# Masks of both tiles as signs from ScalarE in a top-k attention with a gated product

## The chip, the cores and the metric

The kernel runs on one core of one Trainium2 chip. The metric is device microseconds of that core, the median of several runs. Lower is better. Engines are named as in the profile: PE is TensorE (PEld its weight loads), ACT is ScalarE, DVE is VectorE, POOL is GpSimd, SP is SyncE, which issues most DMAs. All times are microseconds (us) unless marked ns.

## What is computed

Attention over 4 x 8 heads with 576 rows of 64 columns. Each row of scores keeps only its 32 largest entries; the others are masked before the softmax. The result, 2304 tokens of 512 columns, then goes through a gated product of two matrices and an output matrix.

```python
B, H, S, D = q.shape          # 4, 8, 576, 64
scores = (1.0 / np.sqrt(D)) * np.matmul(q, k.transpose(0, 1, 3, 2))
kth = np.partition(scores, -32, axis=-1)[..., -32:-31]
scores = np.where(scores >= kth, scores, -1000000000.0)
scores = scores - np.max(scores, axis=-1, keepdims=True)
attn = np.exp(scores)
attn = attn / (np.sum(attn, axis=-1, keepdims=True) + 1e-09)
attn_out = np.matmul(attn, v)
x = attn_out.transpose(0, 2, 1, 3).reshape(B * S, H * D)
out = (x @ w_a) * (x @ w_b) @ w_out   # 512 -> 1536 -> 512
```

## The kernel before

**Units.** The attention is cut into 72 units. A unit is 128 query rows of two heads (a pair), or, for the last 64 rows of the sequence, 64 rows of each of four heads (a tail unit). Its scores are two tiles, j = 0 and 1, of 128 x 576 float32, in `scores[:, u % 3, j, :]`. Four units make the 128 tokens of a group, 18 groups in all. The gated product of a group is made in four chunks of 384 of the 1536 inner columns, so there are 72 chunks too, and chunk n runs in step s = n + 5. All products are made of high and low parts (three matmuls for one), which is why copies, differences and `_hi`, `_lo` tiles are everywhere.

**Steps.** Each engine runs a hand-written program with a loop over steps s, and semaphores tie the programs together. Nothing is reordered: an engine that waits holds all that is written behind it. In step s a unit is in each stage of a pipeline:

- PE: `probs_v(s-2)` (L557), scores of unit s+1 (`qk`, L523), half of the columns of chunk n (L588), transposition of the hidden tile (`turn_hidden`, L599), nine transpositions of the normalised scores of unit s-1 (`transposes`, L539: four for tile 0, five for tile 1), transposed keys and queries, `output(n-2)` (L620), the other half of the columns of chunk n (L588). For each first chunk of a group (n % 4 == 0) a part of the first half is made behind the transpositions (`late_blocks`).
- ACT: in this order `exps(s-1)` for both tiles (L724, two ACTIVATEs with sums), `guard` (L732, the sums plus epsilon), in one of four steps `copy_y` (L793), `x_out(s-2)` (L759, L762), `copy_ab(n-1, 1)` (L773), the scores of unit s+1 out of PSUM (L702, two halves) with `normalise(s-1)` (L739) behind each half, `copy_probs_t(s-1)` (L747, L749), `mask_sign(s)` (L715), `copy_q(s+3)` (L692, L694), `copy_hidden(n-1)` (L780, L782), `copy_ab(n, 0)` (L773, in the first chunk of a group it stands behind the guard of the next step instead), and in 12 steps (four for each of the batches 1 to 3: steps 10, 12, 15, 16, 28, 30, 32, 34, 46, 48, 51, 52) `copy_k` (L678, L682), the keys of a coming pair.
- POOL: `negate(s-1)` (L882), which makes `neg`, the negated scaled maximum and the negated scaled 32nd value of each row, from `best`; `masked(s-1, 0)` and `masked(s-1, 1)` (L901), which add `keep` to the scores; `split_k` (L866) in the steps of keys; `hidden_lo(n-2)` (L917), `hidden(n-1)` (L908), `low_of_x`, `split_q`.
- DVE: the search for the 32 largest of both tiles of unit s. Four rounds of MAX8 (`find`, L976), with MATCH_REPLACE8 between them (`take_out`, L993). The reciprocal of the sums of unit s-1 (`invert`, L1003) stands behind the second `take_out`. At the unit's end comes the comparison with the 32nd value, `below` (L1008), which writes -3e38 where a score is lower and 0 elsewhere into `keep[:, j, :]`.

**Two ways to a mask.** In units 0 to 9 DVE compares for both tiles. From unit 10 (`SIGN0`) it compares for tile 0 alone, and ACT makes the mask of tile 1: `mask_sign` takes the sign of (score - 32nd value) as int8 into the highest byte of each float of `keep`, which held -3e38. A negative sign gives a byte of all ones, so the float is about -3e38 again; 0 and +1 give a float near zero. A memset in unit 10 (L1031) sets the floats up once, and `s_keep` tells ACT of it. The addition on POOL waits for `keep_ready[j]`.

Of the kernel before, what the change touches and what calls it, by code (L numbers as in the profile page):

```python
# [6 lines left out]
def topk_attention_gated_product(nc, q, k, v, w_parts, xs, out):  # L7
    fp32, fp32r, int8 = mybir.dt.float32, mybir.dt.float32r, mybir.dt.int8
    ALU, ACT = mybir.AluOpType, mybir.ActivationFunctionType

    P = 128
    BH, S, D = q.shape
    TOPK = 32
    ROUNDS = TOPK // 8
    SCALE = 1.0 / D ** 0.5
    NEG = -3.0e38
# [32 lines left out]
    ROWS = 3  # L49
# [35 lines left out]
    for n in range(KB, NPREPS):  # L85
        b, p, old = n // KB, n % KB, n - KPAIRS
# [52 lines left out]
    with ExitStack() as ctx:  # L139
        def sb(name, shape, dt=fp32):  # L140
            return ctx.enter_context(nc.sbuf_tensor(name, shape, dt))

        def sem(name):
            return ctx.enter_context(nc.semaphore(name))
# [16 lines left out]
        scores = sb("scores", [P, ROWS, 2, S])  # L161
        work = sb("work", [P, 2, S])
        keep = sb("keep", [P, 2, S])
        best = sb("best", [P, 2, 2, TOPK])

        neg = sb("neg", [P, 2, 2, 2])
# [14 lines left out]

        keep_sign = keep[:].rearrange("p j c -> p (j c)").bitcast(int8).rearrange("p (j c b) -> p j c b", j=2, b=4)[:, 1, :, 3]

        ps = ctx.enter_context(nc.psum_tensor("ps", [P, 8, 512], fp32))

# [65 lines left out]
        s_keep = sem("s_keep")  # L253
# [28 lines left out]
        keep_ready = [sem("keep0_ready"), sem("keep1_ready")]  # L282
        mask_done = sem("mask_done")
# [24 lines left out]
        def unit(u):  # L308
            return 0 <= u < NU
# [347 lines left out]
        def _(act):  # L657
            A = nc.scalar
# [5 lines left out]
            def weights(s, m):  # L664
                for i in w_of(s, m):
                    split_hi(i)
# [38 lines left out]
                act.wait_ge(qk_done, 2)  # L705
                A.copy(scores[:, 0, j, :].rearrange("p (a c) -> p a c", a=2), ps[:, j:j + 3:2, 0:HALF]).then_inc(s_ready, 1)  # L706

            def mask_sign(u):
                if not unit(u) or u < SIGN0:
                    return  # L710
                act.wait_ge(neg_ready, u + 1)
                if u == SIGN0:
                    act.wait_ge(s_keep, 1)
                act.wait_ge(mask_done, 2 * (u - 1) + 2)
                A.activation(keep_sign, scores[:, u % ROWS, 1, 0:S], ACT.Sign, bias=neg[:, u % 2, 1, 1:2], scale=SCALE  # L715
                             ).then_inc(keep_ready[1], 1)

            def exps(u, j):
                if not unit(u):
# [31 lines left out]
            def x_out(u):  # L751
                if not unit(u):
                    return
                b, t, pairs, place = UNITS[u]
                g, at = columns(u)
                act.wait_ge(pv_done, u + 1)
                if g >= 2:
                    wait(act, ab_done[1], NH * (g - 1))
                A.copy(x_hi[:, g % 2, pairs[0]:pairs[-1] + 1, at:at + P // len(pairs)],  # L759
                       ps_x.rearrange("p (j c) -> p j c", j=len(pairs))).then_inc(xhi_done, 1)  # L760
                wait(act, xlo_done, u)
                A.copy(x_raw[:], ps_x).then_inc(xraw_done, 1)  # L762
# [41 lines left out]
            for s in range(FIRST, MOE_END):  # L804
                n = s - MOE0
                if s == NU:
                    x_out(s - 2)
                exps(s - 1, 0)
                exps(s - 1, 1)
                guard(s - 1)  # L810
                if late_blocks(n - 1):
                    copy_ab(n - 1, 0)
                if s >= NU:
                    copy_ab(n - 1, 1)
                if s != NU + 2:
                    copy_y(n - 3)
                weights(s, 0)
                if s != NU:
                    x_out(s - 2)
                if s < NU:  # L820
                    copy_ab(n - 1, 1)
                copy_scores(s + 1, 0)
                weights(s, 1)
                normalise(s - 1, 0)
                copy_scores(s + 1, 1)
                weights(s, 2)
                normalise(s - 1, 1)
                copy_probs_t(s - 1, 0)
                copy_probs_t(s - 1, 1)
                mask_sign(s)  # L830
                copy_q(s + 3)
                weights(s, 3)
                copy_hidden(n - 1)
                if not late_blocks(n):
                    copy_ab(n, 0)
                for m in preps_at(s):
                    copy_k(m)
                weights(s, 4)
                if s == NU + 1:
                    copy_y(n - 2)  # L840
# [105 lines left out]
        @block.vector  # L946
        def _(dve):
            V = nc.vector
            count = 1

            V.memset(k_rows[TAIL:P, :, FULL, :, :], 0.0).then_inc(s_kpad, 1)
            V.memset(work[:], 0.0).then_inc(chain, 1)
            dve.wait_ge(chain, 1)
            for n in range(2):
                V.tensor_copy(q_t[:, n, :, :], work[:, :, 0:6 * D]).then_inc(s_qzero, 1)
            dve.wait_ge(qhi_ready, 1)
            dve.wait_ge(q_copied, 1)
            V.tensor_tensor(q_columns(0, 1), q_whole[:].rearrange("p (b c) -> p b c", b=2), q_columns(0, 0),
                            ALU.subtract).then_inc(qt_ready, 1)
            dve.wait_ge(khi_ready, 1)  # L960
            V.tensor_tensor(k_t[:, 0, 1, :], keys_in_psum(0)[0][0][:, 0:S], k_t[:, 0, 0, :], ALU.subtract
                            ).then_inc(klo_first, 1)
            for h in range(2):
                rows = slice((1 - h) * TAIL, (2 - h) * TAIL)
                ins = V.memset(v_rows[rows, :, TAILS, h * D:(h + 1) * D], 0.0)
            ins.then_inc(s_vpad, 1)

            def find(u, r):
                nonlocal count
                for j in range(2):  # L970
                    if r > 0:
                        dve.wait_ge(chain, taken[j])
                    elif u == 0:
                        dve.wait_ge(s_ready, j + 1)
                    src = scores[:, u % ROWS, j, 0:S] if r == 0 else work[:, j, :]
                    ins = V.max(best[:, u % 2, j, 8 * r:8 * r + 8], src)  # L976
                    if r == ROUNDS - 1:
                        ins.then_inc(kth_ready, 1)
                    elif r == 0:
                        ins.then_inc(max_ready, 1)  # L980
                    else:
                        ins.then_inc(chain, 1)
                        count += 1
                        found[j] = count

            def take_out(u, r, j):
                nonlocal count
                src = scores[:, u % ROWS, j, 0:S] if r == 0 else work[:, j, :]
                if r == 0:
                    dve.wait_ge(max_ready, 2 * u + j + 1)  # L990
                else:
                    dve.wait_ge(chain, found[j])
                V.match_replace(out=work[:, j, :], in_to_replace=best[:, u % 2, j, 8 * r:8 * r + 8],  # L993
                                in_values=src, imm_value=NEG).then_inc(chain, 1)
                count += 1
                taken[j] = count

            def invert(u):
                if not unit(u):
                    return  # L1000
                dve.wait_ge(eps_ready, u + 1)
                wait(dve, p_ready, 2 * (u - 2) + 2)
                V.reciprocal(inverse[:, u % 2, :], sums_eps[:]).then_inc(inv_ready, 1)  # L1003

            def below(u, j):
                dve.wait_ge(kth_ready, 2 * u + j + 1)
                wait(dve, mask_done, 2 * (u - 1) + j + 1)
                V.tensor_scalar(keep[:, j, :], scores[:, u % ROWS, j, 0:S], best[:, u % 2, j, TOPK - 1:TOPK], NEG,  # L1008
                                ALU.is_lt, ALU.mult).then_inc(keep_ready[j], 1)

            found, taken = [0, 0], [0, 0]
            for s in range(NU):
                if s > 0:
                    dve.wait_ge(s_ready, 2 * s + 2)
                find(s, 0)
                take_out(s, 0, 0)
                take_out(s, 0, 1)
                find(s, 1)
                take_out(s, 1, 0)
                take_out(s, 1, 1)  # L1020
                invert(s - 1)
                find(s, 2)
                take_out(s, 2, 0)
                take_out(s, 2, 1)
                find(s, 3)
                below(s, 0)
                if s < SIGN0:
                    below(s, 1)
                elif s == SIGN0:
                    dve.wait_ge(mask_done, 2 * s)  # L1030
                    V.memset(keep[:, 1, :], NEG).then_inc(s_keep, 1)  # L1031
            invert(NU - 1)

# [28 lines left out]
```

## Time and profile before

| | |
|---|---|
| median of 3 runs | 818.16 us (817.97 to 818.72) |
| the profiled execution's own time | 817.8 us |
| its span, first to last instruction | 815.4 us |
| PE busy | 771.7 us (95%) |
| DVE busy | 744.3 us (91%) |
| ACT busy | 657.0 us (81%) |
| POOL busy | 507.4 us (62%) |
| mean granted PE clock | 0.98 |

Busy time is the time in which at least one instruction of the engine runs. A matmul is pipelined and its end is modelled: one of 384 columns is listed with some 340 ns and the next starts about 175 ns after it. So a busy PE may still have short holes, and starts say more than durations. ACT and DVE instructions overlap a little too. A bracket behind a row of the timeline is the idle time of the engine before that instruction, and what ended it.

### The profile page before, as it was taken

The numbers are of one execution on the slowest core, as the hardware profiler recorded it, in microseconds if no ns is written. First come the engines' busy times: TensorE is split into PE (matmuls) and PEld (weight loads), VectorE is DVE, ScalarE is ACT, GpSimd is POOL, SyncE is SP. The second block draws the span as 40 slices with busy tenths as digits, with TensorE's granted clock in tenths as the row PEclk, the third lists the DMA queues.
The fourth block names the chain that finished last, engine by engine and source line by source line (L and its number), as shares of the span: only waits on it lengthen the run. The fifth ranks groups of instructions, "written<-read, shape, count | busy, mean of one in ns | idle before, by whom it ended". The sixth has DMA issues, their size and how long they took to land.

```text
span 815.4 us, 18431 instructions
## 1 busy us (share of the span) xinstructions
PE 771.7 (95%) x5952; PEld 686.3 (84%) x5952; DVE 744.3 (91%) x1603; ACT 657.0 (81%) x1614; POOL 507.4 (62%) x560
## 2 busy tenths in 40 slices
PE   5368899999999999999999999999999999999998
PEld 4246788899998989898889899989998889898887
DVE  6999999998999999999999999999999999999500
ACT  5678978888888888888888888888888888888732
POOL 2989986656555666666756565665656555665532
PEclk9957999999999999999999999999999999999999
DMA  6566754445553444444644443544463434343562
GB/s 169 150 186 199 217 185 148 138 137 150 149 167 113 140 125 129 126 138 142 178 142 134 128 137 122 145 136 136 137 183 123 137 124 137 124 133 117 167 214 84
DMA packets 117245, 119.16 MB, mean 146 GB/s; under 512 B 61856, under 2 KB 80288, under 8 KB 117152
## 3 DMA queue, kind: packets, MB, share of 16 engines
q1 hardware_dynamic: 116880, 117.93, 47.8%
q8 instruction: 50, 0.82, 0.4%
q14 instruction: 43, 0.35, 0.2%
q10 hardware_dynamic: 272, 0.07, 0.0%
HBM read 108.53 MB, written 9.44 MB: 145 GB/s over the span
## 4 chain that ended last, share of the span: by engine, by line
PE 86%; POOL 5%; DVE 4%; DMA 2%; issue 2%; ACT 1%; SPq 0%; POOLq 0%; ACTq 0%
PE ps L588 37%; PE ps L620 18%; PE ps L557 10%; PE ps L523 9%; PE ps L539 8%; PE ps L599 3%; DVE best L976 2%; DVE work L993 2%; POOL scores L901 2%; POOL w_lo L856 1%; POOL k_t L856 1%; DMA x_scratch<-k_t 1%; PE ps L492 1%; PE ps L501 1%; DMA stage<-in_w 0%
## 5 line engine op out<-in xcount | busy, mean ns | idle before, releaser
L976 DVE MAX8 best<-work 128x8 f32<-128x576 f32 x432 | 304.4, 747 | 0.0
L901 POOL TENSOR_TENSOR scores<-scores,keep 128x576 f32<-128x576 f32 x144 | 207.0, 1441 | 37.4 <-ACT keep L715 36.6
L993 DVE MATCH_REPLACE8 work<-best,work 128x576 f32<-128x576 f32 x288 | 212.0, 745 | 0.0
L588 PE MATMUL ps<-w_hi,x_hi 128*128 128x384 f32 x576 | 202.5, 351 | 2.4 <-issue 1.2
L588 PE MATMUL ps<-w_hi,x_lo 128*128 128x384 f32 x576 | 194.4, 338 | 0.0
L908 POOL TENSOR_TENSOR ab<-ab 128x384 f32<-128x384 f32 x72 | 73.3, 1018 | 158.6 <-ACT ab L773 158.6
L588 PE MATMUL ps<-w_lo,x_hi 128*128 128x384 f32 x432 | 145.8, 337 | 0.0
L747 ACT COPY probs_t<-ps 128x512 f32<-128x512 f32 x144 | 82.2, 586 | 51.8 <-PE ps L539 49.7
L588 PEld LDWEIGHTS ps<-w_hi,x_hi 128*128 128x128 f32 x576 | 108.1, 188 | 17.5 <-issue 13.9
L724 ACT ACTIVATE scores<-scores,neg 128x576 f32<-128x576 f32 x144 | 114.4, 822 | 6.6 <-POOL scores L901 6.4
L739 ACT ACTIVATE scores<-scores,inverse 128x576 f32<-128x576 f32 x144 | 115.4, 803 | 0.3 <-DVE inverse L1003 0.3
L539 PE MATMUL ps<-ident,scores 128*128 128x128 f32 x648 | 90.1, 283 | 26.2 <-ACT scores L702 19.2
L588 PEld LDWEIGHTS ps<-w_hi,x_lo 128*128 128x128 f32 x576 | 108.1, 188 | 0.0
L993 DVE MATCH_REPLACE8 work<-best,scores 128x576 f32<-128x576 f32 x144 | 106.0, 745 | 0.0
L976 DVE MAX8 best<-scores 128x8 f32<-128x576 f32 x144 | 101.9, 750 | 2.5 <-ACT scores L706 2.5
L539 PEld LDWEIGHTS ps<-ident,scores 128*128 128x128 f32 x648 | 74.7, 145 | 33.5 <-ACT scores L739 17.8
L557 PE MATMUL ps<-probs_t,v_rows 128*64 128x128 f32 (+1 forms) x1600 | 99.5, 274 | 2.5 <-ACT probs_t L749 2.5
L557 PEld LDWEIGHTS ps<-probs_t,v_rows 128*64 128x64 f32 x1600 | 82.3, 141 | 21.0 <-issue 16.9
L702 ACT COPY scores<-ps 128x576 f32<-128x576 f32 x142 | 93.4, 658 | 2.0 <-PE ps L523 1.9
L620 PE MATMUL ps<-w_hi,h_hi 128*128 128x512 f32 x216 | 91.1, 422 | 0.5 <-issue 0.4
L523 PE MATMUL ps<-k_t,q_t 64*128 64x288 f32 x960 | 87.6, 319 | 3.3 <-ACT k_whole L682 1.9
L588 PEld LDWEIGHTS ps<-w_lo,x_hi 128*128 128x128 f32 x432 | 81.3, 188 | 3.0
(64 smaller groups left out, 1300.9 us busy)
## 6 DMA issues: line engine op xcount, KB each, us to landing
wo_lo<-x_scratch SPq DMA_DIRECT2D x69, 768.0 KB, 4.5
wb_lo<-x_scratch SPq DMA_DIRECT2D x70, 384.0 KB, 4.1
stage<-in_w SPq DMA_DIRECT2D x36, 256.0 KB, 3.1
x_scratch<-k_t SPq DMA_DIRECT2D x18, 256.0 KB, 2.4
k_rows<-in_k SPq DMA_DIRECT2D x32, 128.0 KB, 4.7
v_rows<-in_v SPq DMA_DIRECT2D x32, 128.0 KB, 2.6
out<-stage SPq DMA_DIRECT2D x16, 256.0 KB, 4.2
q_rows<-in_q SPq DMA_DIRECT2D x63, 64.0 KB, 3.5
```

Of the source, the lines that this page charges most:

```text
L523: last = mm(ps_s[half][:, j, :], q_t[rows, u % 2, qpart, first:first + 2 * D], k_t[rows, (b * KB + p) % KPAIRS, kpart, at:at + HALF], star ...
L539: last = tr(to, row_of(u)[:, at:at + P], ident[:])
L557: last = mm(ps_x[h * D:(h + 1) * D, i * w:(i + 1) * w], v_rows[:, p, block, h * D:(h + 1) * D], probs_t[:, at:at + w], start=(i == 0 and c ...
L588: last = mm(ps_ab[which], x[:, g % 2, kb, :], w, start=(kb == 0 and m == 0), stop=(kb == KB - 1 and m == 2))
L620: last = mm(ps_y, x[:, cols], w, start=(f + b == 0 and m == 0), stop=(f + b == NF - 1 and m == 2))
L702: A.copy(scores[:, u % ROWS, :, half * HALF:(half + 1) * HALF], ps_s[half]).then_inc(s_ready, 1)
L724: A.activation(row, row, ACT.Exp, bias=neg[:, u % 2, j, 0:1], scale=SCALE, accum_out=sums[:, u % 2, j:j + 1]).then_inc(e_ready, 1)
L739: A.mul(row, row, inverse[:, u % 2, j:j + 1]).then_inc(p_ready, 1)
L747: A.copy(probs_t[:, a:a + FULL * P], ps[:, 2 + j, :]).then_inc(pt_ready, 1)
L901: V.tensor_tensor(row, row, keep[:, j, :], ALU.add).then_inc(mask_done, 1)
L976: ins = V.max(best[:, u % 2, j, 8 * r:8 * r + 8], src)
L993: V.match_replace(out=work[:, j, :], in_to_replace=best[:, u % 2, j, 8 * r:8 * r + 8], in_values=src, imm_value=NEG).then_inc(chain, 1)
```

## The change

From unit 10 on, `keep_sign` covers both tiles, and `mask_sign(s, j)` is called for j = 0 and j = 1, one behind the other, at the place where the call for tile 1 stood. Each waits for the negated values of its unit and for the addition that last read its half of `keep`. DVE makes no comparison from unit 10 on, and in unit 10 its memset covers both halves. The first addition on POOL now waits for ACT's first sign, the second for the second. All else is as it was. One line more in ACT's loop moves the line numbers of what stands behind it by one.

```diff
@@ -181,7 +181,7 @@
-        keep_sign = keep[:].rearrange("p j c -> p (j c)").bitcast(int8).rearrange("p (j c b) -> p j c b", j=2, b=4)[:, 1, :, 3]
+        keep_sign = keep[:].rearrange("p j c -> p (j c)").bitcast(int8).rearrange("p (j c b) -> p j c b", j=2, b=4)[:, :, :, 3]
 
         ps = ctx.enter_context(nc.psum_tensor("ps", [P, 8, 512], fp32))
 
@@ -705,15 +705,15 @@
                 act.wait_ge(qk_done, 2)
                 A.copy(scores[:, 0, j, :].rearrange("p (a c) -> p a c", a=2), ps[:, j:j + 3:2, 0:HALF]).then_inc(s_ready, 1)
 
-            def mask_sign(u):
+            def mask_sign(u, j):
                 if not unit(u) or u < SIGN0:
                     return
                 act.wait_ge(neg_ready, u + 1)
                 if u == SIGN0:
                     act.wait_ge(s_keep, 1)
-                act.wait_ge(mask_done, 2 * (u - 1) + 2)
-                A.activation(keep_sign, scores[:, u % ROWS, 1, 0:S], ACT.Sign, bias=neg[:, u % 2, 1, 1:2], scale=SCALE
-                             ).then_inc(keep_ready[1], 1)
+                act.wait_ge(mask_done, 2 * (u - 1) + j + 1)
+                A.activation(keep_sign[:, j, :], scores[:, u % ROWS, j, 0:S], ACT.Sign, bias=neg[:, u % 2, j, 1:2], scale=SCALE
+                             ).then_inc(keep_ready[j], 1)
 
             def exps(u, j):
                 if not unit(u):
@@ -827,7 +827,8 @@
                 normalise(s - 1, 1)
                 copy_probs_t(s - 1, 0)
                 copy_probs_t(s - 1, 1)
-                mask_sign(s)
+                mask_sign(s, 0)
+                mask_sign(s, 1)
                 copy_q(s + 3)
                 weights(s, 3)
                 copy_hidden(n - 1)
@@ -1023,12 +1024,12 @@
                 take_out(s, 2, 0)
                 take_out(s, 2, 1)
                 find(s, 3)
-                below(s, 0)
                 if s < SIGN0:
+                    below(s, 0)
                     below(s, 1)
                 elif s == SIGN0:
                     dve.wait_ge(mask_done, 2 * s)
-                    V.memset(keep[:, 1, :], NEG).then_inc(s_keep, 1)
+                    V.memset(keep[:], NEG).then_inc(s_keep, 1)
             invert(NU - 1)
 
 # ---- launch ----
```

On ACT, unit 11, from the transposed probabilities to the copies of queries (`keep` is the mask, `neg` the negated values):

```order
 L747 COPY probs_t<-ps 128x512 x2
 L749 COPY probs_t<-ps 128x128
-L715 ACTIVATE keep<-scores,neg 128x576
+L715 ACTIVATE keep<-scores,neg 128x576 x2
 L692 CAST q_t<-ps 128x128
 L694 COPY q_whole<-ps 128x128
```

Two ACTIVATEs stand where one stood, ahead of the copies of the queries.

On DVE, a unit behind unit 10, from the reciprocal to the first search of the next unit, before:

```order
L1003 RECIPROCAL inverse<-sums_eps 128x2
L976 MAX best<-work 128x8 x2
L993 MATCH_REPLACE work<-best,work 128x576 x2
L976 MAX best<-work 128x8 x2
L1008 TENSOR_SCALAR keep<-scores,best 128x576
L976 MAX best<-scores 128x8 x2
```

and now, where L976 has become L977:

```order
L1004 RECIPROCAL inverse<-sums_eps 128x2
L977 MAX best<-work 128x8 x2
L994 MATCH_REPLACE work<-best,work 128x576 x2
L977 MAX best<-work 128x8 x2
L977 MAX best<-scores 128x8 x2
```

The TENSOR_SCALAR between the last search of a unit and the first of the next is gone.

## Rows read from the trace of the kernel before

**Rows 1.** By stretches: window, its length, busy us (and instructions) of PE, PEld, DVE, ACT, POOL; clock.
```profile
120.00:770.00 650.00, 649.05 (x5176) 582.77 (x5175) 630.52 (x1365) 550.55 (x1362) 398.31 (x447) 1.00 0.46 137
```

**Rows 2.** Waits of 120 to 770 us: who waited for whom; us in total, times, longest.
```profile
ACT x_hi L759 <- PE ps L557: 45.9, 51, 2.8
DVE inverse L1003 <- ACT sums_eps L732: 14.2, 15, 1.8
PEld ps L539 <- issue: 2.2, 7, 0.3
PEld ps L539 <- ACT scores L739: 1.3, 7, 0.2
```

**Rows 3.** Timeline of ACT and POOL, a plain step: start, us, engine, line, operation, operands.
```profile
465.04 0.97 ACT L715 ACTIVATE keep<-scores,neg 128x576 int8<-128x576 f32 x1
...
465.86 0.25 ACT L692 CAST q_t<-ps 128x128 fp32r<-128x128 f32 x1
...
468.04 0.81 ACT L724 ACTIVATE scores<-scores,neg 128x576 f32<-128x576 f32 x1
...
468.96 0.20 ACT L732 ACTIVATE sums_eps<-sums 128x2 f32<-128x2 f32 x1
...
469.96 0.27 ACT L759 CAST x_hi<-ps 128x128 fp32r<-128x128 f32 x1 [0.31 <-PE ps L557]
...
472.37 0.82 ACT L739 ACTIVATE scores<-scores,inverse 128x576 f32<-128x576 f32 x1
...
466.08 1.44 POOL L901 TENSOR_TENSOR scores<-scores,keep 128x576 f32<-128x576 f32 x1 [0.33 <-ACT keep L715]
```

**Rows 4.** Timeline of PE, the same step and the start of the next transpositions.
```profile
472.88 0.34 PE L588 MATMUL ps<-w_hi,x_lo 128*128 128x384 f32 x1
473.05 0.49 PE L599 MATMUL ps<-ident,ab 128*128 128x128 f32 x3
473.38 1.15 PE L539 MATMUL ps<-ident,scores 128*128 128x128 f32 x9
...
483.51 1.15 PE L539 MATMUL ps<-ident,scores 128*128 128x128 f32 x9
```

**Rows 5.** Timeline of ACT and PE, a step whose transpositions come early.
```profile
449.64 0.27 ACT L759 CAST x_hi<-ps 128x128 fp32r<-128x128 f32 x1 [0.77 <-PE ps L557]
...
452.06 0.81 ACT L739 ACTIVATE scores<-scores,inverse 128x576 f32<-128x576 f32 x1
...
452.52 1.17 PE L539 MATMUL ps<-ident,scores 128*128 128x128 f32 x9
```

**Rows 6.** Timeline of ACT, the start of a group of tokens.
```profile
454.37 0.96 ACT L715 ACTIVATE keep<-scores,neg 128x576 int8<-128x576 f32 x1
...
457.06 0.78 ACT L724 ACTIVATE scores<-scores,neg 128x576 f32<-128x576 f32 x1
...
459.81 0.27 ACT L759 CAST x_hi<-ps 128x128 fp32r<-128x128 f32 x1 [1.28 <-PE ps L557]
```

**Rows 7.** Timeline of ACT and PE after a key preparation, first kind.
```profile
513.99 0.80 ACT L739 ACTIVATE scores<-scores,inverse 128x576 f32<-128x576 f32 x1
...
514.51 1.15 PE L539 MATMUL ps<-ident,scores 128*128 128x128 f32 x9
```

**Rows 8.** Timeline of PE after a key preparation, second kind.
```profile
139.05 1.35 PE L539 MATMUL ps<-ident,scores 128*128 128x128 f32 x9
```

**Rows 9.** Timeline of ACT and PE after a key preparation, third kind.
```profile
203.32 0.80 ACT L739 ACTIVATE scores<-scores,inverse 128x576 f32<-128x576 f32 x1
...
204.14 1.15 PE L539 MATMUL ps<-ident,scores 128*128 128x128 f32 x9
```

**Rows 10.** Groups of DVE's instructions, and its and POOL's timeline across a search.
```profile
L1008 DVE TENSOR_SCALAR keep<-scores,best 128x576 f32<-128x576 f32 x62 | 31.3, 505 | 0.0
...
511.02 0.17 DVE L1003 RECIPROCAL inverse<-sums_eps 128x2 f32<-128x2 f32 x1 [0.70 <-ACT sums_eps L732]
...
515.37 0.41 POOL L882 TENSOR_SCALAR neg<-best 128x4 f32<-128x4 f32 x1 [0.99 <-DVE best L976]
```

## The prediction

> **What bounds the kernel now.** The page's busy shares come first: three engines lie close together, so shares over the span don't choose. The table by stretches is next [rows 1]: from 120 to 770 us, which is where the change acts (unit 10 onwards), a matmul is in flight in 649.05 of 650 us at full clock, VectorE is busy for 630.52 us (97%), ScalarE for 550.55 (85%). The table of waits says for whom [rows 2]: VectorE waited 14.2 us, 15 times, for ScalarE's sums. The stops of TensorE's stream that stand out in the stretch are seven in front of the transpositions (L539), 2.2 and 1.3 us in all, which waited for ScalarE's normalise (L739). ScalarE in turn waits for TensorE once per step at `x_out` (45.9 us, 51 times [rows 2]). So TensorE sets the pace at about 10.13 us a step (its transpositions start at 473.38 and 483.51 [rows 4]); VectorE's work is nearly as long, and ScalarE has a reserve that differs from step to step. The question is where a second sign finds room in it.
>
> A busy row of pipelined matmuls can hide short holes, so I looked at starts: the last matmul of 384 columns starts at 472.88, the next instruction at 473.05 [rows 4], 0.17 us later, and this distance stands between all of L588's matmuls in the steps that I read, whether VectorE waits in them or not. I take it that the stream has no holes. The Trainium skill (Perfetto Trace Analysis, Identifying the Most-Contended Engine) warns that matmul busy time overstates TensorE and asks for the share of weight loads. That share is 582.77 of 650 us here [rows 1], 90%, under VectorE's 97%: by that rule VectorE is the engine to relieve, the change would pay, and this is the first rival's case. The Trainium skill (Perfetto Trace Analysis, Optimizing Scalar/DVE Operations) also suggests handing work to ScalarE when VectorE is full.
>
> **The change, part by part.**
> (1) *VectorE loses the comparison (L1008) of 62 units*, 505 ns each [rows 10], 31.3 us in all. VectorE will wait longer for `s_ready` and for the sums; since TensorE doesn't wait for it, this is worth nothing. The single memset of `keep` in unit 10 becomes twice as wide (once, about half a microsecond, in place of a comparison as long): nothing.
>
> (2) *ScalarE takes 62 more signs.* One takes 0.97, but the next instruction starts 0.82 after it (465.04 to 465.86 [rows 3]), so ScalarE moves back by 0.82 us per step. The work between it and the next wait is `copy_q`, `copy_hidden`, `copy_ab`, the exponentials and the guard. The Trainium skill (ScalarE: Activation LUTs, What ACT_TABLE_LOAD costs) gives about 280 ns + 0.833 ns per element for an activation with a pointer bias and an overlap of 93 ns, so an estimate of 0.67 in place of 0.82; the sum at the end would be about 5.3 instead of 7.7 us. The row is of the very instruction, so it decides.
>
> (3) *The addition of mask 0 on GpSimd now follows a sign.* Before, it started right after the negation (L882) and ran beside the sign. Now both additions follow: 0.97 of the first sign, 0.07 of handoff (the sign ends at 466.01, the addition starts at 466.08 [rows 3]) and 1.44 + 1.44 make 3.92 us from the start of the first sign until the second tile may be exponentiated. In a plain step the second exponential starts 3.00 us after the sign (468.04 [rows 3]), now 3.82, so it waits 0.1 more. Where a new group of tokens starts, ScalarE copies one product less ahead of it: 457.06 - 454.37 = 2.69 [rows 6], now 3.51, so it waits 0.42 more.
>
> (4) *What of this reaches TensorE, by kind of step.* A delay is swallowed first by the wait at `x_out`, then by the distance from the end of the second normalise to the fifth transposition, which reads it (some 0.44 us after the first starts: all nine, overlapped, take 1.15 [rows 4]).
> - Plain steps: delay 0.82 + 0.1 = 0.92. Where `copy_y` is in the step the wait is 0.31 [rows 3], 0.61 is left; the normalise ends at 473.19 and is read at 473.82 [rows 3, 4], a distance of 0.63. The two are equal within the reading, so I take 0.03 for each of seven steps: 0.2 us. Where the wait is 0.77 and the distance 0.6, nothing.
> - Steps whose transpositions come early, since fewer matmuls stand ahead of them: wait 0.77, so 0.15 to 0.17 is left; the normalise ends at 452.87 and is read at 452.96 [rows 5], distance 0.09. Nine steps (two of them with the last tile, whose wait is a little longer and whose distance is nil), 0.08 each: 0.7 us.
> - Group starts: wait 1.28 [rows 6] against 0.82 + 0.42 = 1.24. Nothing, with no reserve left.
> - Key preparations, 12 of them (four for each of three batches). The copies of keys stand between the sign and `x_out`, and ScalarE's wait there is gone already or under 0.15 us and then covered by GpSimd's split of the same keys, which moves back too. So all of 0.82 arrives. In five of them TensorE waits already (nine transpositions take 1.35 us in place of 1.15 [rows 4, 8]): 5 x 0.82 = 4.1 us. In three the distance is 514.95 - 514.79 = 0.16 [rows 7]: 3 x 0.66 = 2.0. In two it is 204.58 - 204.12 = 0.46 [rows 9]: 2 x 0.36 = 0.7. In the last two TensorE has twice the score products to do ahead of it, the distance is larger than 0.82: nothing.
>
> A delay doesn't pile up, since ScalarE waits for TensorE again at `copy_probs_t` in each step; but what TensorE stood still is never won back, because it is the engine that is full. Sum: 4.1 + 2.0 + 0.7 + 0.7 + 0.2 = **7.7 us**. Against the profiled execution (817.8 us, span 815.4) that is 825.5; the median of the runs is 0.36 higher, so **825.9 us**. From below: if half of the delay in preparation steps is found again (VectorE earlier, so inverse and negation earlier), 3.5 us, 821.7. From above: handoffs of 0.05 to 0.1 us that I took as nothing, in some 25 tight steps, add up to 2 us, and group starts that have no reserve some tenths each for 13: 830.
>
> **The rivals.**
> *VectorE was the bound (faster).* For it: in 47 of the 62 units VectorE didn't wait at all [rows 2], so its own step is as long as TensorE's. With 31 us taken off, the time would be 787. Against it: TensorE's starts leave no room. A weaker form holds at most the seven stops: 2.2 + 1.3 = 3.5 us, 814.7. Together 0.08, nearly all of it for the weaker form.
>
> *Absorbed (no change).* ScalarE's order leaves a hole in the preparation steps that I don't see, for example since the inverse is ready earlier. Then about 818.2. Against: ScalarE's rows in those steps are back to back from the sign to `x_out`. 0.10.
>
> *The ring of the mask becomes the pace (much slower).* Sign, two additions, second exponential, guard, reciprocal, the rest of VectorE's search, negation, next sign now form a ring: 3.92 up to the second exponential, 1.12 from its start to the guard's end (468.04 to 469.16 [rows 3]), 4.35 from the reciprocal (511.02) to the negation (515.37), 0.41 for the negation [rows 10], and some 0.1 of handoffs: 9.9 us, against 10.13 of TensorE. Before, its first part ran beside VectorE's own work. It decides if it is 0.25 us longer than I add up, for example by 0.05 at each of its five handoffs. At 10.4 us a step it would cost 0.27 x 50 = 13 us on top of part of the sum: 836. 0.12.
>
> That the comparison isn't gone, or the signs aren't added, is ruled out by the order of instructions.
>
> **How the numbers follow.** Forecast 0.70, ring 0.12, absorbed 0.10, faster 0.08. Faster by over 0.2% (about 1.6 us, what a measurement of this kernel tells from no change): 0.08. Within it: 0.10. Slower: 0.82. The range starts at 818.5, which leaves out the faster case and part of the absorbed one, and goes to 833, which takes in the upper bound of the forecast (830) and the ring if it is only just over.
>
> **What would show it.** In the profile after: the comparison 20 times, the sign 124 times at 0.97; VectorE's wait for `sums_eps` up from 14 us to 50 or more and a new one for `s_ready`; ScalarE's wait at `x_hi` down from 45.9 to under 15 us, its wait at `probs_t` also lower. TensorE's waits ahead of L599 and L539 up by about 7 us, nearly all in the ten preparation steps named, each about 0.4 to 0.8; busy ScalarE 700 to 715 us. I am wrong if the normalise isn't what TensorE waits for, if stops of the same size stand in plain steps (the ring; GpSimd's negation would then be followed by the sign at once, with ScalarE waiting for `neg`), or if TensorE's step falls under 10.1 us (the first rival).

## Result

The changed kernel takes **824.77 us** (median of 4 runs, 824.53 to 825.0) beside 818.07 us (817.77 to 818.72) of the kernel before. The ratio is 1.0081, with a 95% interval of 1.0063 to 1.0098: slower by 6.7 us. The forecast was 825.9 us, 7.7 us more than before. (One run of all that follow, one of experiment 8, took 960.2 us at a mean granted clock of 0.74 and is left out.)

The profiled execution took 824.83 us with a span of 823.0, against 817.8 and 815.4. From the page of after, busy time by engine:

```profile
PE 772.7 (94%) x5952; PEld 684.6 (83%) x5952; DVE 720.8 (88%) x1541; ACT 707.3 (86%) x1676; POOL 493.7 (60%) x560
```

ScalarE is busy for 50 us more and VectorE for 23.5 us less (744.3 before), TensorE for nearly as long as before. (VectorE's comparisons were 31.3 us; its searches and removals take 753 ns each in this profile, against 747 and 745, and so give some of it back.) The waits of 120 to 778 us answer to [rows 2]; the columns are who waited for whom, us in total, times, longest:

```profile
POOL scores L902 <- ACT keep L715: 107.7, 62, 3.0
...
DVE inverse L1004 <- ACT sums_eps L732: 45.4, 52, 2.3
ACT probs_t L747 <- PE ps L539: 33.8, 50, 1.4
...
PEld ps L599 <- issue: 6.9, 12, 1.0
...
PEld ps L539 <- issue: 3.8, 12, 0.3
PE ps L599 <- issue: 3.4, 6, 0.7
PEld ps L539 <- ACT scores L739: 2.3, 12, 0.2
ACT x_hi L759 <- PE ps L557: 1.5, 3, 0.6
```

ScalarE's wait at `x_out`, 45.9 us before, is down to 1.5: that is the reserve that the second sign has eaten. VectorE's wait for the sums went from 14.2 to 45.4 us: that is where its comparisons went. TensorE's stops right ahead of the transpositions (L539) went from 7 to 12. Those one group earlier, ahead of `turn_hidden` (L599), grew more: its weight loads stop for 6.9 us, 12 times, where the kernel before had 0.9 us, 3 times. `issue` at L599 means that the profile shows no releaser. In the program `turn_hidden` waits for the product of the hidden tile on GpSimd, and the product for ScalarE's `copy_ab`.

**Where the 7.6 us of span are.** I compared the start of the first transposition of every step in both traces. These are the rows of after for steps 10, 54 and 70:

```profile
127.70 0.49 PE L539 MATMUL ps<-ident,scores 128*128 128x128 f32 x3
...
598.63 1.15 PE L539 MATMUL ps<-ident,scores 128*128 128x128 f32 x9
...
761.80 1.15 PE L539 MATMUL ps<-ident,scores 128*128 128x128 f32 x9
```

and of before:

```profile
127.67 0.49 PE L539 MATMUL ps<-ident,scores 128*128 128x128 f32 x3
...
590.95 1.15 PE L539 MATMUL ps<-ident,scores 128*128 128x128 f32 x9
...
754.11 1.15 PE L539 MATMUL ps<-ident,scores 128*128 128x128 f32 x9
```

The shift is 0.03 us at step 10, 7.68 at step 54 and 7.69 at step 70. All of it comes from the stretch with key preparations; the sixteen steps from 54 to 70 add 0.01. In between it comes in jumps (the part that falls into the next step's distance is added), with what the prediction had:

| steps behind a key preparation | predicted each | measured each | sum |
|---|---|---|---|
| 11, 13, 29, 33, 49 | 0.82 | 1.09, 0.78, 0.78, 0.79, 0.79 | 4.2 (4.1) |
| 31, 35, 47 | 0.66 | 0.73, 0.72, 0.73 | 2.2 (2.0) |
| 17, 53 | 0.36 | 0.75, 0.47 | 1.2 (0.7) |
| 16, 52 | 0 | 0.00, 0.00 | 0 |
| nine steps with early transpositions | 0.08 | at most 0.03 | 0 (0.7) |
| seven steps with `copy_y` | 0.03 | at most 0.03 | 0 (0.2) |

The starts of the same matmuls, compared one by one, also say where in the step TensorE loses the time. Of the 7.6 us, 4.4 are lost ahead of `turn_hidden`, 1.6 between it and the first transposition, 1.0 from there to the end of the nine, and 0.6, in step 11 alone, at the products with the values and the scores (L557, L523, of which 0.37 is a wait for ScalarE's copied keys, L682). In steps 13, 29, 33 and 49 nearly all of the jump stands ahead of `turn_hidden`, as in step 13 of after:

```profile
159.34 0.48 ACT L773 COPY ab<-ps 128x384 f32<-128x384 f32 x1 [0.56 <-POOL h_lo L918]
...
159.96 1.01 POOL L909 TENSOR_TENSOR ab<-ab 128x384 f32<-128x384 f32 x1 [0.73 <-ACT ab L773]
...
161.07 0.52 PE L599 MATMUL ps<-ident,ab 128*128 128x128 f32 x3 [0.57 <-issue]
161.71 1.35 PE L539 MATMUL ps<-ident,scores 128*128 128x128 f32 x9
```

and of before:

```profile
157.47 0.48 ACT L773 COPY ab<-ps 128x384 f32<-128x384 f32 x1 [0.34 <-POOL h_lo L917]
...
159.25 0.49 PE L599 MATMUL ps<-ident,ab 128*128 128x128 f32 x3
159.84 1.35 PE L539 MATMUL ps<-ident,scores 128*128 128x128 f32 x9
```

Late keys from ScalarE make GpSimd's `split_k` and `hidden_lo` late, ScalarE's copy of `ab` waits for these, and GpSimd's product and TensorE's `turn_hidden` follow. The product ends at 160.97 and `turn_hidden` starts at 161.07. The transpositions take 1.35 us in both kernels.

Step 47 shows the other kind. ACT of after, from the signs to the second normalise, and PE from `turn_hidden` on ([rows 7] before):

```profile
511.32 1.76 ACT L715 ACTIVATE keep<-scores,neg 128x576 int8<-128x576 f32 x2
512.93 0.26 ACT L692 CAST q_t<-ps 128x128 fp32r<-128x128 f32 x1
...
517.25 0.20 ACT L732 ACTIVATE sums_eps<-sums 128x2 f32<-128x2 f32 x1
...
517.82 0.27 ACT L759 CAST x_hi<-ps 128x128 fp32r<-128x128 f32 x1
...
520.46 0.79 ACT L739 ACTIVATE scores<-scores,inverse 128x576 f32<-128x576 f32 x1
...
520.10 0.52 PE L599 MATMUL ps<-ident,ab 128*128 128x128 f32 x3
520.72 1.35 PE L539 MATMUL ps<-ident,scores 128*128 128x128 f32 x9
```

Two signs and the next start take 1.61 (511.32 to 512.93). No bracket stands behind any row of ScalarE from there to the second normalise, so nothing is swallowed. The normalise ends at 521.25, and the nine transpositions take 1.35 us in place of 1.15 because the fifth waits for it. Of this step's 0.73 us, 0.24 are lost ahead of `turn_hidden`, 0.29 between it and the first transposition (which in the program waits for the second half of the next scores, L702, copied by 520.57), and 0.20 from the fifth on. So three pieces of ScalarE's work hold TensorE one behind the other, and the last of them, the normalise, sets how late the step ends.

### The profile page after: what moved, and what is told of

It reads as the page before. It is cut to its first block, busy times and chain, and to the rows that moved or that the text cites. A ratio compares the mean times of both kernels' runs of the same rounds, so it can differ in the third digit from the quotient of the medians.

```text
span 823.0 us, 18431 instructions
## 1 busy us (share of the span) xinstructions
PE 772.7 (94%) x5952; PEld 684.6 (83%) x5952; DVE 720.8 (88%) x1541; ACT 707.3 (86%) x1676; POOL 493.7 (60%) x560
## 4 chain that ended last, share of the span: by engine, by line
PE 86%; POOL 4%; DVE 4%; issue 2%; DMA 2%; ACT 1%; SPq 0%; POOLq 0%; ACTq 0%
PE ps L588 37%; PE ps L620 18%; PE ps L557 10%; PE ps L523 8%; PE ps L539 8%; PE ps L599 3%; DVE best L977 2%; DVE work L994 2%; POOL scores L902 1%; POOL w_lo L857 1%; PE ps L492 1%; PE ps L501 1%; POOL k_t L857 1%; DMA stage<-in_w 1%; DMA x_scratch<-k_t 1%
## 5 line engine op out<-in xcount | busy, mean ns | idle before, releaser
L977 DVE MAX8 best<-work 128x8 f32<-128x576 f32 x432 | 305.7, 753 | 0.0
L539 PE MATMUL ps<-ident,scores 128*128 128x128 f32 x648 | 90.2, 282 | 29.1 <-ACT scores L702 21.7
L715 ACT ACTIVATE keep<-scores,neg 128x576 int8<-128x576 f32 x124 | 109.1, 952 | 1.1 <-POOL neg L883 1.1
L539 PEld LDWEIGHTS ps<-ident,scores 128*128 128x128 f32 x648 | 73.7, 144 | 38.1 <-ACT scores L739 19.6
L977 DVE MAX8 best<-scores 128x8 f32<-128x576 f32 x144 | 101.6, 752 | 2.6 <-ACT scores L706 2.6
L557 PE MATMUL ps<-probs_t,v_rows 128*64 128x128 f32 (+1 forms) x1600 | 99.4, 274 | 2.6 <-ACT probs_t L749 2.5
L557 PEld LDWEIGHTS ps<-probs_t,v_rows 128*64 128x64 f32 x1600 | 82.3, 141 | 21.2 <-issue 17.0
L702 ACT COPY scores<-ps 128x576 f32<-128x576 f32 x142 | 93.4, 659 | 1.2 <-PE ps L523 1.1
L523 PE MATMUL ps<-k_t,q_t 64*128 64x288 f32 x960 | 85.7, 314 | 3.4 <-ACT k_whole L682 2.3
```

The source lines that it names most:

```text
L523: last = mm(ps_s[half][:, j, :], q_t[rows, u % 2, qpart, first:first + 2 * D], k_t[rows, (b * KB + p) % KPAIRS, kpart, at:at + HALF], star ...
L539: last = tr(to, row_of(u)[:, at:at + P], ident[:])
L557: last = mm(ps_x[h * D:(h + 1) * D, i * w:(i + 1) * w], v_rows[:, p, block, h * D:(h + 1) * D], probs_t[:, at:at + w], start=(i == 0 and c ...
L702: A.copy(scores[:, u % ROWS, :, half * HALF:(half + 1) * HALF], ps_s[half]).then_inc(s_ready, 1)
L715: A.activation(keep_sign[:, j, :], scores[:, u % ROWS, j, 0:S], ACT.Sign, bias=neg[:, u % 2, j, 1:2], scale=SCALE).then_inc(keep_ready[j], 1)
```

## Experiments

All ratios are against runs of the kernel before on the same chip. The theory: the cost is ScalarE's time in the preparation steps, and VectorE's relief is worth nothing.

**1. VectorE compares for tile 0 in the preparation units.** The diff against the changed kernel; VectorE's comparison writes the same byte as the sign:

```diff
+    def signs(u):
+        if u < SIGN0:
+            return ()
+        return (1,) if preps_at(u) else (0, 1)
...
-                if not unit(u) or u < SIGN0:
+                if not unit(u) or j not in signs(u):
                     return
...
+            def below_byte(u, j):
+                dve.wait_ge(kth_ready, 2 * u + j + 1)
+                dve.wait_ge(mask_done, 2 * (u - 1) + j + 1)
+                if u == SIGN0:
+                    dve.wait_ge(s_keep, 1)
+                V.tensor_scalar(keep_sign[:, j, :], scores[:, u % ROWS, j, 0:S], best[:, u % 2, j, TOPK - 1:TOPK], -1.0,
+                                ALU.is_lt, ALU.mult).then_inc(keep_ready[j], 1)
...
+                if s >= SIGN0:
+                    for j in range(2):
+                        if j not in signs(s):
+                            below_byte(s, j)
```

> Two signs from ScalarE in 50 of the 62 units; in the 12 units whose step prepares keys VectorE compares for tile 0 again (it writes the same byte, -1 or 0, into keep) and ScalarE signs tile 1 alone. Theory (the loss is 0.82 us of ScalarE in the ten tight preparation steps, the other steps swallow it): 818.1 us, between 817.3 and 819.2. Rival (the ring of sign, additions, exponential, reciprocal and search, or the additions on GpSimd that now follow the sign, costs a little in every step): at least 821, since 50 of 62 units keep it.

817.77 us, ratio 0.9999 (0.9990 to 1.0009). Fifty units with two signs cost nothing that can be measured.

**2. Two signs in the preparation units alone.** Experiment 1 with one line changed:

```diff
-        return (1,) if preps_at(u) else (0, 1)
+        return (0, 1) if preps_at(u) else (1,)
```

> The complement: two signs in the 12 units of the preparation steps alone, in the other 50 one sign and a comparison of tile 0 on VectorE. Theory: the whole loss is here, 824.8 us, between 823.8 and 825.5. Rival (a cost in every step): under 821. If this and the run before it don't add up to the whole change, the units of the two kinds act on each other.

824.29 us, ratio 1.0076 (1.0061 to 1.0091). Twelve units carry the loss, and within the intervals the two halves add up to the whole (1.0081). The jumps are those of the table within 0.03, save at step 11 (0.69 here) and step 17 (0.47).

The traces say what the rest of step 11 is. The first two signs, in unit 10, wait for the memset that sets `keep` up. The bracket behind them names GpSimd's negation, but that had ended at 129.80. Before:

```profile
129.83 0.54 DVE L1031 MEMSET keep<- 128x576 f32 x1
...
130.46 0.95 ACT L715 ACTIVATE keep<-scores,neg 128x576 int8<-128x576 f32 x1 [0.84 <-POOL neg L882]
```

and after, twice as wide:

```profile
129.68 1.02 DVE L1032 MEMSET keep<- 128x1152 f32 x1 [0.19 <-issue]
...
130.78 1.75 ACT L715 ACTIVATE keep<-scores,neg 128x576 int8<-128x576 f32 x2 [1.14 <-POOL neg L883]
```

The sign starts 0.32 us later, 0.29 beyond TensorE's shift of 0.03 at that time, and 0.79 + 0.29 = 1.08 stands beside the 1.09 of the table. Experiment 2 has the same memset, but there TensorE came to step 10 0.6 us later than in the kernel before, and step 11 lost less. In general step 11 depends on when the start-up lets TensorE arrive: it begins step 10's transpositions between 127.3 and 129.9 us in the fourteen profiles, and where it comes late enough (2.2 us later, in experiment 6) step 11 has no stop at all; in experiment 8, where it is 1.7 us later, the two signs make no jump in it. In step 17 the extra 0.28 us stands ahead of `turn_hidden`: ScalarE's copy of `ab` starts 0.39 us after GpSimd's low part of the hidden tile has ended, where it is 0.11 in the other preparation steps and in experiment 2. What held this one copy is open.

**3. One more sign, VectorE keeps its comparisons.** Against the kernel before:

```diff
+        spare = sb("spare", [P, S], int8)
...
+            def spare_sign(u):
+                if not unit(u) or u < SIGN0:
+                    return
+                act.wait_ge(neg_ready, u + 1)
+                A.activation(spare[:], scores[:, u % ROWS, 1, 0:S], ACT.Sign, bias=neg[:, u % 2, 1, 1:2], scale=SCALE)
...
+                spare_sign(s)
                 mask_sign(s)
```

> The kernel before with one more sign per unit from unit 10, of tile 1 into a tile that nobody reads; VectorE keeps its comparison of tile 0, and the addition of mask 0 starts right after the negation as before. It separates ScalarE's time from the order of the masks and from VectorE's relief. Theory (ScalarE's time alone): 824.8 us, 824.0 to 825.8. Rival one (the additions, now behind the sign, are the cost): 818 to 820. Rival two (VectorE's relief did gain something that the sign ate): slower than the changed kernel by 2 us or more, 827 and up.

819.53 us, ratio 1.0018 (1.0009 to 1.0028). By the expectation this was the verdict for the first rival, and it was wrong. The profile shows jumps behind the same preparations as in the changed kernel, only smaller (0.66 to 0.68 at steps 13, 29, 33 and 49, since this sign costs 0.67 from start to start), save at step 11, which has none. But the steps between them were shorter than before. The long matmuls followed each other at 173 ns instead of 175. The one thing left that could do this was the new tile: it had moved every tile allocated behind `keep` by 576 bytes. Experiments 5 and 6 take the two apart.

**4. No mask for tile 0.** Against the kernel before, VectorE's half of the change alone:

```diff
-                below(s, 0)
                 if s < SIGN0:
+                    below(s, 0)
                     below(s, 1)
...
-                pool.wait_ge(keep_ready[j], u + 1)
+                pool.wait_ge(keep_ready[j], min(u + 1, SIGN0) if j == 0 else u + 1)
```

> The other half alone: VectorE makes no comparison from unit 10 on and ScalarE has its one sign. Tile 0 is masked with what the comparison of unit 9 left, so the computation of tile 0's mask is left out from unit 10. Theory: VectorE's 31 us are worth nothing, 818.1 us, 817.3 to 818.6. Rival (VectorE is the engine that binds, or its lateness makes the seven stops of TensorE): 814.7 or less.

817.96 us, ratio 0.9998 (0.9989 to 1.0008). Taking 31 us of work from VectorE, the engine that is busy for 91% of the span, changed nothing. VectorE turned them into waiting, in this run's stretch of 120 to 770 us (14.2 before):

```profile
DVE inverse L1003 <- ACT sums_eps L732: 37.1, 41, 2.4
...
PEld ps L539 <- issue: 2.2, 7, 0.3
PEld ps L539 <- ACT scores L739: 1.3, 7, 0.2
```

TensorE's seven stops are as they were, so VectorE doesn't cause them either.

**5. The spare sign with its tile behind all others.** As experiment 3, but for the place of the tile:

```diff
         h_lo = sb("h_lo", [P, HC], fp32r)
+        spare = sb("spare", [P, S], int8)
```

> The spare sign again, with its tile behind all other tiles in SBUF, so that none of them moves (in the first form 576 bytes stood ahead of eleven tiles, and TensorE's matmuls of 384 columns then followed each other at 173 ns in place of 175). Its sign costs 0.67 us from start to start, since it writes packed bytes. Theory (ScalarE's time alone makes the stops, and the first form was faster by the layout): 5 x 0.67 + 3 x 0.5 + 2 x 0.25 = 5.3, so 823.0 us, 822.3 to 824. Rival (the order of masks is most of the cost): 819.5 again.

822.88 us, ratio 1.0059 (1.0044 to 1.0074). ScalarE's time alone makes the stops, with VectorE's comparisons and GpSimd's order of masks as before. 5.3 us were expected by the prediction's own sum, 4.9 came. The agreement is in part luck: step 11, for which 0.67 were expected, has no jump here either (TensorE comes to step 10 0.8 us later), and the others add up to 5.1.

**6. The kernel before with 576 unused bytes behind `keep`.**

```diff
         keep = sb("keep", [P, 2, S])
+        spare = sb("spare", [P, S], int8)
```

> The kernel before with nothing but the 576 bytes that nobody uses, ahead of the eleven tiles, as in the first form of the spare sign. If the layout speeds the matmuls up: 815.3 us, 814.5 to 816.5, and 173 ns between matmuls. If the faster matmuls came from the sign's own doing: 818.1.

814.27 us, ratio 0.9955 (0.9940 to 0.9970). An unused tile makes the kernel 3.7 us faster. The first transpositions of steps 38 and 42, four steps without a stop between them, in this kernel:

```profile
422.58 1.15 PE L540 MATMUL ps<-ident,scores 128*128 128x128 f32 x9
...
463.00 1.15 PE L540 MATMUL ps<-ident,scores 128*128 128x128 f32 x9
```

and in the kernel before:

```profile
422.61 1.15 PE L539 MATMUL ps<-ident,scores 128*128 128x128 f32 x9
...
463.21 1.15 PE L539 MATMUL ps<-ident,scores 128*128 128x128 f32 x9
```

Four steps take 40.42 us here and 40.60 there, 0.4% less, with the same instructions and no wait in either.

**7. VectorE compares for both tiles in the preparation units,** elsewhere VectorE compares for tile 0 and ScalarE signs tile 1, as before. Experiment 1 with one line changed:

```diff
-        return (1,) if preps_at(u) else (0, 1)
+        return () if preps_at(u) else (1,)
```

> The kernel before, but in the 12 units whose step prepares keys VectorE compares for both tiles and ScalarE signs none; ScalarE has 0.82 us less there. Theory (ScalarE's lateness in preparation steps is what stops TensorE, in the kernel before too): five of its seven stops of about 0.5 us go, 815.7 us, 815.2 to 816.8. Rival (VectorE's extra 0.45 in those units delays the negation or the inverse instead): 818 or more.

816.1 us, ratio 0.9978 (0.9968 to 0.9987), faster than the kernel before. The seven stops of [rows 2] are four, with 1.2 and 0.8 us in place of 2.2 and 1.3:

```profile
PEld ps L544 <- issue: 1.2, 4, 0.3
...
PEld ps L544 <- ACT scores L744: 0.8, 4, 0.2
```

Five were expected to go, and three went (steps 29, 33 and 49). Those of steps 11 and 13 stayed, shorter by 0.08 and 0.07 us. In step 13 GpSimd is the late engine: VectorE ends its search late, the negation starts at 152.06 us where it was 150.28 (TensorE is only 0.6 us behind by then), and GpSimd works without a pause from there to the low part of the hidden tile. So the expectation's rival holds there.

**8. The ring made longer.** The changed kernel, with a comparison whose result is not used in front of VectorE's last search; the tile is behind all others:

```diff
                 take_out(s, 2, 1)
+                if s >= SIGN0:
+                    V.tensor_scalar(spare[:], scores[:, s % ROWS, 0, 0:S], 1.0, 1.0, ALU.is_lt, ALU.mult)
                 find(s, 3)
```

> The changed kernel with one comparison more on VectorE in each unit from 10, between the third removal and the last search, so that the ring (sign, additions, exponential, guard, reciprocal, search, negation) is longer by about 0.45 us; its result is not used. In the changed kernel the negation ends 0.03 us ahead of the sign in one unit of four and about 0.5 ahead in the others. If the ring is as tight as the prediction has it (it decides from 0.25 us on): 0.2 x 50 us more, 834 to 836. If a late sign is swallowed by the distances behind it as well: 825 to 827.

825.33 us, ratio 1.0088 (1.0068 to 1.0108), against 1.0081 for the changed kernel. The ring did close: ScalarE now waits for the negated values (120 to 770 us),

```profile
ACT keep L716 <- POOL neg L884: 2.3, 9, 0.3
```

and in 26 of the 62 units the negation ends 0.03 to 0.07 us ahead of the sign. It costs nothing that can be measured: from step 12 to step 54 TensorE loses 6.6 us against the kernel before in both, and from 54 to 70 nothing in both. These waits, 0.3 us at the longest, are swallowed before they reach TensorE.

**9. Both improvements together.** Experiment 7 with the 576 bytes of experiment 6.

> Both things that were faster than the kernel before, together: VectorE compares for both tiles in the 12 preparation units, and the 576 unused bytes stand behind keep. If they are independent: 818.0 - 1.9 - 3.7 = 812.4 us, 811.8 to 813.2. If one hides the other: 814 or more.

**811.74 us, ratio 0.9920 (0.9907 to 0.9934).** The best version: 6.4 us faster than the kernel before.

**10 to 12. Which tile's place it is.** Three kernels, each with one unused tile: 576 bytes directly ahead of `x_hi` (10), 576 directly ahead of `ab` (11), and 64 ahead of `x_hi` (12). The comments behind # are not in the kernels:

```diff
+        spare = sb("spare", [P, S], int8)      # 10; [P, 64] in 12
         x_hi = sb("x_hi", [P, 2, KB, G], fp32r)
         x_lo = sb("x_lo", [P, 2, KB, G], fp32r)
+        spare = sb("spare", [P, S], int8)      # 11
         ab = sb("ab", [P, 2, HC])
```

> The kernel before with the 576 unused bytes directly ahead of x_hi, so that only x_hi, x_lo, ab, h_hi and h_lo move and probs_t, best, neg and the sums stay. If it is the address of what TensorE loads as weights or of what is copied into them: 814.3 us. If it is the address of probs_t or the small tiles: 818.0.

813.32 us, ratio 0.9945 (0.9931 to 0.9958).

> The same bytes directly ahead of ab, so that only ab, h_hi and h_lo move and x_hi, x_lo stay. If x_hi and x_lo are what matters, 818.0 us; if h_hi and h_lo (the output's matmuls got faster too, 9 of 33 long matmuls a step), about 817; if all five share it, in between.

817.55 us, ratio 0.9993 (0.9984 to 1.0002). This is not quite without effect: from 120 to 770 us the output's matmuls of 512 columns, whose weights are `h_hi` and `h_lo`, followed each other at 230.3 ns in place of 232.4 (means from the starts), and those of 384 columns at 180.8 in place of 180.3 (median 175 in both). The two nearly cancel out.

> The kernel before with only 64 unused bytes ahead of x_hi. 576 bytes are nine times 64, so modulo 128 the tiles move by the same 64 bytes. If the place of x_hi and x_lo within 128 bytes is what matters: 813.5 us, 812.8 to 815. If it is the larger distance: 818.0.

814.03 us, ratio 0.9951 (0.9934 to 0.9967).

So the gain comes when `x_hi` and `x_lo`, which TensorE loads as weights, move too, and 64 bytes are enough. No run moved these two alone: in 10 and 12 `ab`, `h_hi` and `h_lo` move with them, and the matmuls of 512 columns are faster as well (229.7 ns in both). Whether it is the reading by TensorE or the writing by ScalarE and GpSimd, and which residue of the address counts, was not tried.

## Why the prediction was right

- *TensorE is the bound, VectorE is not.* Right: experiment 4 gives VectorE's half of the change as 0.9998. The Trainium skill (Perfetto Trace Analysis, Identifying the Most-Contended Engine) would have chosen VectorE by the 90% of weight loads beside its 97% [rows 1], if the share of peak arithmetic, for which it asks as well, is left aside. Here the runs speak against that rule, and the distance between starts was the better sign.
- *A sign costs ScalarE 0.82 us from start to start.* Right: 512.93 - 511.32 = 1.61 for two. The Trainium skill's figure (ScalarE: Activation LUTs, What ACT_TABLE_LOAD costs), an estimate of 0.67, holds for the packed output of experiments 3 and 5; the mask's output has a stride of four bytes and takes 0.15 more.
- *The loss comes behind the key preparations alone, by three kinds.* Right in place and, in sum, in size (7.6 of span for a predicted 7.7; the medians differ by 6.7, the two profiled executions by 7.0, since the time outside the span was 2.4 us before and is 1.8 after, which the prediction took as unchanged). That the sum fits this closely is in part luck: terms of 0.9 us were nil, while step 11 (the wide memset, priced at nothing, cost 0.3) and steps 17 and 53 were larger than priced. Experiments 1 and 2 split the change at just this line: 0.9999 and 1.0076.
- *The way by which the delay reaches TensorE.* Half right. The prediction lets it arrive at the fifth transposition, which waits for the normalise, and that is still the last gate: in the steps of the first kind it waits as long as before, 1.35 us for nine in both kernels. But TensorE stands elsewhere. 4.4 of the 7.6 us are lost one group earlier, at `turn_hidden`, by way of the copy of `ab` and the product (in steps 13, 17, 29, 33 and 49 GpSimd's split of the keys and its low part stand in this way too), and the sum has no such gate. It came out all the same because everything behind the signs is late by the same 0.8 us, whichever gate TensorE meets first. By the prediction's own words ("I am wrong if the normalise isn't what TensorE waits for") this part was not right, though its signs named L599 as well.
- *The small terms of the plain steps, 0.7 and 0.2 us, were too large: they are nil.* The step that failed is the size of the reserve at `x_out`. I took the bracket as all of it. But ScalarE's instructions overlap by some 0.1 us: in the kernel before `x_hi` could have started at about 448.78, when the guard (448.67) was 0.11 old, so the reserve was 0.86 and not 0.77. In the changed kernel the guard and `x_hi` follow each other at exactly this distance, and the delay ends there:

```profile
450.37 1.76 ACT L715 ACTIVATE keep<-scores,neg 128x576 int8<-128x576 f32 x2
...
454.28 0.78 ACT L724 ACTIVATE scores<-scores,neg 128x576 f32<-128x576 f32 x1
...
455.18 0.20 ACT L732 ACTIVATE sums_eps<-sums 128x2 f32<-128x2 f32 x1
455.29 0.26 ACT L759 CAST x_hi<-ps 128x128 fp32r<-128x128 f32 x1
```

  `x_hi` starts 5.65 us later than before (449.64 [rows 5]), and TensorE's transpositions of this step 5.67 later, 458.19 against 452.52, as much as TensorE was late already. The term of steps 17 and 53 was too small in turn, 0.7 for 1.2.
- *GpSimd's additions behind the sign.* Right: they run back to back behind ScalarE's first sign, as this row of GpSimd's timeline shows. ScalarE's exponentials wait for them for 7.3 us in 18 waits from 120 to 778 us (1.4 us, 2 waits before), and by experiment 1 this costs nothing that can be measured.

```profile
471.74 2.84 POOL L902 TENSOR_TENSOR scores<-scores,keep 128x576 f32<-128x576 f32 x2 [2.05 <-ACT keep L715]
```

  The second exponential starts 3.91 us after the sign (450.37 to 454.28), where 3.92 were worked out.
- *The ring as a rival.* Its length was about right (the negation ends 0.03 to 0.04 us ahead of the sign in 8 of the 62 units), but the point from which it decides was not: 0.25 us on paper, while about 0.45 more on VectorE moved the time by 0.6 us at most (experiment 8).
- *Signs in the profile.* The reciprocal's wait rose, to 45.4 us where 50 or more were said, and `x_hi`'s fell under 15. A wait of VectorE for `s_ready` was forecast and did not come: VectorE waits at the reciprocal, and by its next unit the scores are there.

## What to carry over

When three engines are nearly full, ask for each kind of step where the late engine's delay would be swallowed, and price the change in the steps that swallow nothing: here 12 units of 62 carried all of it, and an assignment by unit (VectorE compares for both tiles where keys are prepared, elsewhere ScalarE signs one of the two) beat both kernels. List everything that the bound engine takes from the late one in a step: here it met three such gates, and the first of them, not the one in the sum, took most of the time. Read the reserve of an engine from starts, since the bracket of idle time is short by what its instructions overlap (0.77 against 0.86 us here). And give an added tile a place behind all others, or measure its bytes alone: an experiment that moves addresses measures two things.

## What the runs showed of the hardware

Moving `x_hi` and `x_lo`, which TensorE loads as weights, and the three tiles behind them by 64 bytes in SBUF changed the distance between its matmuls of 384 columns from about 175 to 173 ns, at the same granted clock (1.00 in the stretch), and the whole kernel by 0.5% (818.21 to 814.03 us). Moving only `ab`, `h_hi` and `h_lo` left the kernel as it was (ratio 0.9993). A sign of 128 x 576 elements that writes bytes at a stride of four takes 965 ns and holds the next instruction for 0.82 us; with packed bytes it is 788 ns and 0.67 us.
